# Attention and two dense stages in fp32r on one core: the key blocks of the row maximum, from 384, 384, 384 to 512, 512, 128 columns

## The reference

```python
def _attn_ref(q, k, v):
    B, H, S, D = q.shape                      # 4, 8, 1152, 64
    q_pool = q.reshape(B, H, S // 2, 2, D).mean(axis=3)
    scores = 1.0 / np.sqrt(D) * np.matmul(q_pool, k.transpose(0, 1, 3, 2))
    scores = scores - np.max(scores, axis=-1, keepdims=True)
    attn = np.exp(scores)
    attn = attn / (np.sum(attn, axis=-1, keepdims=True) + 1e-09)
    return np.matmul(attn, v)

def _moe_ref(x, w_in, w_out):                 # 512 -> 2048 -> 512
    h = x @ w_in
    return (h * (1.0 / (1.0 + np.exp(-h)))) @ w_out

def _moe2_ref(x, w1, w2, w3, w_out):          # 512 -> 1024 -> 1024 -> 512
    return (((x @ w1) * (x @ w2)) @ w3) @ w_out
```

## Time and profile before

| | us |
|---|---|
| median of 3 runs | 1342.31 |
| the profiled execution | 1341.67 |
| its span in the trace | 1339.6 |
| TensorE busy | 1292.4 (96%) |
| VectorE busy | 592.4 (44%) |
| ScalarE busy | 599.6 (45%) |
| GpSimd busy | 342.5 (26%) |

### The profile page before, as it was taken

The page is one execution under the profiler, slowest core; times in us unless marked ns, Lnnn a source line. Parts: engine busy times, 40 slices in busy tenths (PEclk is TensorE's granted clock), DMA queues, the critical chain, the costliest instruction groups (busy, mean ns, idle before and its releaser), DMA issues.

```text
span 1339.6 us, 26046 instructions
## 1 busy us (share of the span) xinstructions
PE 1292.4 (96%) x10896; PEld 1151.2 (86%) x10896; DVE 592.4 (44%) x886; ACT 599.6 (45%) x1114; POOL 342.5 (26%) x295
## 2 busy tenths in 40 slices
PE   6999999999999999999999999999999999999998
PEld 4999999999999999988888888888998888888888
DVE  6777777777767777733311112111136222222221
ACT  3666666667666666673322222222245121212211
POOL 4556565665656565440000000000000000000000
PEclk9999999999999999999999999999999999999999
DMA  4122222221121211102100000000125000000001
GB/s 136 47 70 71 72 71 72 72 71 49 60 72 54 71 58 50 36 27 64 48 8 1 1 0 1 0 0 0 48 88 180 0 1 32 0 32 0 32 9 40
DMA packets 25300, 58.57 MB, mean 44 GB/s; under 512 B 7136, under 2 KB 7776, under 8 KB 25184
## 3 DMA queue, kind: packets, MB, share of 16 engines
q1 hardware_dynamic: 25184, 56.91, 13.2%
HBM read 52.04 MB, written 4.79 MB: 42 GB/s over the span
## 4 chain that ended last, share of the span: by engine, by line
PE 91%; DVE 3%; ACT 3%; issue 2%; DMA 1%; POOL 0%; ACTq 0%; SPq 0%; DVEq 0%
PE psum L875 18%; PE psum L877 18%; PE psum L876 18%; PE psum L942 17%; PE psum L892 9%; PE psum L921 8%; PE psum L923 2%; DVE mx L682 2%; ACT psum L501 1%; DVE pL L716 1%; ACT tmpB L517 1%; PE psum L903 1%; ACT tmpA L516 1%; ACT qH L522 0%; DMA qraw<-in_qT 0%
## 5 line engine op out<-in xcount | busy, mean ns | idle before, releaser
L682 DVE TENSOR_REDUCE mx<-psum 128x2 f32<-128x768 f32 x240 | 228.6, 957 | 95.8 <-PE psum L892 95.8
L496 ACT ACTIVATE pH<-psum 128x576 fp32r<-128x576 f32 x288 | 188.5, 655 | 179.9 <-PE psum L923 178.9
L942 PE MATMUL psum<-pH,vH 64*128 64x288 f32 x1152 | 196.1, 305 | 25.4 <-ACT tmpB L517 23.2
L421 POOL TENSOR_TENSOR pL<-pF,pH 128x576 fp32r<-128x576 f32 x96 | 137.0, 1427 | 227.3 <-ACT pF L499 227.3
L942 PE MATMUL psum<-pH,vL 64*128 64x288 f32 x1152 | 189.1, 292 | 0.0
L942 PE MATMUL psum<-pL,vH 64*128 64x288 f32 x1152 | 188.7, 291 | 0.0
L812 DVE TENSOR_TENSOR gL<-gF,gH 128x512 fp32r<-128x512 f32 (+1 forms) x80 | 51.4, 642 | 305.2 <-ACT gH L587 305.2
L716 DVE TENSOR_TENSOR pL<-psum,pH 128x576 fp32r<-128x576 f32 x192 | 144.5, 752 | 70.6 <-ACT psum L501 69.1
L584 ACT ACTIVATE gF<-psum 128x512 f32<-128x512 f32 (+1 forms) x80 | 44.4, 555 | 266.8 <-PE psum L877 265.5
L942 PEld LDWEIGHTS psum<-pH,vH 64*128 64x128 f32 x1152 | 127.2, 184 | 41.0 <-issue 30.9
L942 PEld LDWEIGHTS psum<-pH,vL 64*128 64x128 f32 x1152 | 127.4, 185 | 0.0
(11 more groups left out here) (96 smaller groups left out, 2702.5 us busy)
## 6 DMA issues: line engine op xcount, KB each, us to landing
qraw<-in_qT SPq DMA_DIRECT2D x16, 576.0 KB, 4.7
kraw<-in_kT SPq DMA_DIRECT2D x16, 576.0 KB, 3.7
vraw<-in_v SPq DMA_DIRECT2D x16, 576.0 KB, 3.8
rsums<-recips SPq DMA_DIRECT2D x32, 144.0 KB, 3.0
wstage<-in_w_in SPq DMA_DIRECT2D x16, 256.0 KB, 4.7
fstage<-in_w3T SPq DMA_DIRECT2D x8, 512.0 KB, 4.9
w12stage<-in_w SPq DMA_DIRECT2D x8, 512.0 KB, 4.6
outT<-oS SPq DMA_DIRECT2D x4, 1024.0 KB, 4.2
```

The costliest lines, as they stand in the source:

```text
L421: pool.tensor_tensor(pL[r][:], pF[n // 3 % 2][:], pH[r][:].bitcast(F32), ALU.subtract).then_inc(pL_pool, 1)
L496: act.activation(pH[r][:], scores, ACT.Exp, scale=SCALE).then_inc(pH_ready, 1)
L682: dve.tensor_reduce(mx[:, qt, :, kb], bank[:, :, 0:KW], AX.X, ALU.max).then_inc(max_taken, 1)
L942: last = pe.matmul(obank[hd], vals[own(rows_of), c, hd:hd + 2, :].rearrange("p e d -> p (e d)"), probs[own(rows_of), hd, :], start=(c == 0 ...
```

## The change

The key blocks become 0 to 511, 512 to 1023 and 1024 to 1151. Items of key blocks 0 and 1 have matmuls of 512 columns, which fill a PSUM bank, and one reduction over 2 x 512 elements. Items of key block 2 have 128 columns and 2 x 128 elements. The order of items and units, and the cut of v, stay. The splits `k_hi` and `k_lo` get the same widths, and the unit they wait for moves from 12, 15, 18 to 13, 17, 18 done of the pair two before.

```diff
-    KW = S // KB
+    KEDGE = (0, 512, 1024, S)
...
         def kblock(b):
-            return slice(b * KW, (b + 1) * KW)
+            return slice(KEDGE[b], KEDGE[b + 1])
+
+        def kwidth(b):
+            return KEDGE[b + 1] - KEDGE[b]
...
             def k_lo(p, b):
                 pool.wait_ge(kH_ready, KB * p + b + 1)
-                need(pool, st_scored, 2 * (UNITS * (p - 2) + NC + CPB * (b + 1)))
+                need(pool, st_scored, 2 * (UNITS * (p - 2) + NC + KEDGE[b + 1] // P))
...
             def k_hi(p, b):
                 act.wait_ge(k_loaded, 16 * (p + 1))
-                need(act, st_scored, 2 * (UNITS * (p - 2) + NC + CPB * (b + 1)))
+                need(act, st_scored, 2 * (UNITS * (p - 2) + NC + KEDGE[b + 1] // P))
...
-                dve.tensor_reduce(mx[:, qt, :, kb], bank[:, :, 0:KW], AX.X, ALU.max).then_inc(max_taken, 1)
+                dve.tensor_reduce(mx[:, qt, :, kb], bank[:, :, 0:kwidth(kb)], AX.X, ALU.max).then_inc(max_taken, 1)
...
-                        last = pe.matmul(bank[:, hd, 0:KW], q[j][own(hd), cols], k[j][own(hd), keys],
+                        last = pe.matmul(bank[:, hd, 0:kwidth(kb)], q[j][own(hd), cols], k[j][own(hd), keys],
                                          start=(s == 0), stop=(s == 2))
```

More of the change, by code:

```diff
@@ L62, in block_kernel @@
     RING = 4
-    assert NC == 9 and Q <= 1024 and KW <= 512 and ITEMS == QT * KB == 15
+    assert NC == 9 and Q <= 1024 and ITEMS == QT * KB == 15
     TILE = 512
```

## The result

The changed kernel takes 1374.11 us (median of 4 runs, 1373.85 to 1374.30) against 1342.70 us (4 runs) beside it: a ratio of 1.0232, 95% interval 1.0214 to 1.0249. It is slower. The forecast was 1375 with a range of 1356 to 1391. The profiled execution's span went from 1339.6 to 1372.2 us, 32.6 more.

A forecast was written before the change was run, and what follows sets the result against it. TensorE bounds it, through a slackless item-reduction-item loop. Per round 2.98 + 0.34 - 1.56 + 0.35 = 2.11 us, by 15 rounds 31.7, plus 1.1 at the start: 1374.4 profiled, so 1375; range 1356 to 1391.

The forecast's parts named there:

- The loop: Item, reduction, item through one pair of PSUM banks sets wide steps: 2.37 us against TensorE's own 2.04.
- The seven loops: Steps after wide items 0, 3, 6, 7, 9, 12 and 13, set by bank reuse: together +2.98 us a round.
- Items with room behind: Wide items with a gap behind: items 1 and 10 pay only columns, +0.17 us each; item 2, before a stall, 0.
- Narrow items: Steps after 128-column items 4, 5 and 8 shorten by 0.28, 0.34 and 0.29 us; item 11, before a stall, 0.
- the reading of `turn_max`: Its nine 64-column matmuls were taken as 0.042 us each, so a 128-column pair was priced at 0.084 us.
- After item 14: `score_t` 16 starts 2.11 us after narrow item 14 in place of 2.76, its low part coming sooner: -0.65 a round.
- The cast: ScalarE's cast of key block 1 runs ahead of exponential 16, delaying item 0: +0.35 us a round, ends 0 and +0.6.
- The start: Pair 0: longer first block, VectorE waits once, about 0.5 us: +1.1 us, between 0.3 and 2.
- rival 1: Waits are absorbed and TensorE pays only columns: +0.35 us a round, 1347 us; chance 0.07.
- rival 2: Faster: wide reductions end within TensorE's own step of 2.04 us, round -0.25, 1338 us; chance 0.04.
- rival 3: Narrow matmuls are dear: a 128-column pair takes 0.21 us, +23 us, 1398 us; chance 0.06.
- rival 4: TensorE's clock falls to half for 3.3 us in each round, costing 25 us: 1400 us; chance 0.03.

The follow-up runs named there:

- the first experiment: The changed kernel, but VectorE reduces only the first 384 columns of each bank of a wide item, matmuls untouched: 1346.88 us, ratio to before 1.0025.

## Why the prediction was right

**The loop.** The mechanism held and the first experiment shows it: with the reduction back at 0.96 us and all matmuls as changed, the kernel is 27 us faster. The seven loops measured +2.71 us a round against the forecast +2.98. I had added to every wide item the 0.83 us lead of an item that had waited. The lead is 0.92 where the first pair was prompt (309.41 to 310.33) and 1.00 where it waited (311.70 to 312.70), so loops that follow a free item are 2.29, not 2.37.

**Items with room behind.** Item 1 +0.17 and item 2 +0.01, as forecast. Items 10 and 11 +0.25 against +0.17. The difference is item 10's first pair: 0.17 us before, when nothing held it, and 0.305 after, 0.07 more than a wide pair costs (0.23), because its bank now comes free late. With the shorter reduction of the first experiment that pair is back at 0.23 and the step 0.07 shorter.

**Narrow items.** This term was mis-sized: the three steps after items 4, 5 and 8 gave 0.68 against 0.91.

The step of the prediction that failed is the reading of `turn_max`. Its 0.38 us for nine matmuls is not an even 0.042 each: in the trace's records the first two pairs start 0.03 us apart (311.75 and 311.78) and the next ones 0.11 apart (311.89, 312.00, 312.11). So a pair of 64 columns costs 0.11 as well, and a pair of 128 costs 0.115 (314.20 to 314.32 to 314.43), not 0.084. The first pair of a narrow item is quick when nothing held it (0.06 in item 5) and takes 0.13 after a wait, and the first `values` pair behind a narrow item takes 0.18 to 0.20 in place of 0.13 (medians). In all, three narrow pairs cost 0.34 us, and 0.41 after a wait, against the 0.25 and 0.32 forecast: the missing 0.08 or so an item.

The 256-column pairs at 0.12 show that this price is nearly flat from 64 to 256 columns. It follows the clock: at a granted clock of 0.50 the pairs of `turn_max` stand 0.21 apart, and its nine matmuls, which before took 0.64 us from first start to last end at 1.00, took 1.24:

```profile
24.82 1.24 PE L906 MATMUL psum<-identR,mneg 64*128 64x64 f32 x9 [2.46 <-DVE mneg L702]
```

The prediction set beside this the estimate of 0.21 us for two weight loads one behind the other, from the Trainium skill's page "TensorE: Matmul & The Clock Gate", section "LDWEIGHTS (loading the stationary operand)". As a sum of two loads it was wrong here, for the loads of the two halves run beside each other (311.86 and 311.88, each 0.19 us long). But the prediction was also wrong to say that the trace disagrees with the page. The 0.042 us is a mean over the loads of both halves, and the page's estimate of 107 ns for one load of 128 columns is close to the 0.11 us that the trace shows between two matmuls of the same half, each with its own load, at full clock. At half clock the same distance is 0.21.

**After item 14.** -0.72 in place of -0.65. `score_t` 16 lost its wait, as forecast, at 2.13 against 2.11; the rest came from its own first pair, which no longer follows a wait (0.53 to `turn_max` in place of 0.63). The narrow last item put in the kernel before shows this gain by itself: 7 us.

**The cast.** +0.27 in place of +0.35, within its ends, and shown from both sides: 3.9 us when it is moved in the changed kernel, 3.7 us when only the split is changed in the old one (0.3 of it in the start). The 0.27 was the part that I had let through to item 0. Before, nothing held item 0 (its first pair took 0.17, and the placing copy had ended 0.37 earlier), so part of the exponential's delay of 0.48 was absorbed. The 0.08 for a slow first pair was counted twice: it does not move item 0's start but shows in the step behind it (2.40, that of an item that waited), and the 2.37 of that step held it already.

**The start** was too low: +1.52 to the first `turn_max` against +1.1. The first reduction came 0.70 later and VectorE waited once, for 0.48, both as forecast:

```profile
9.82 5.72 DVE L685 TENSOR_REDUCE mx<-psum 128x2 f32<-128x1024 f32 x6 [3.03 <-PE psum L895]
16.02 7.87 DVE L685 TENSOR_REDUCE mx<-psum 128x2 f32<-128x1024 f32 x9 [0.48 <-PE psum L895]
```

The other 0.34 is that the 15 reductions fill 13.59 us in place of 13.25. The first wide items start 1.28 us apart (9.55, 10.83, 12.11, 13.39), with pairs 0.43 apart in place of 0.23, slower than VectorE reduces them.

**The first round** cost 1.0 more than the others, which the prediction did not hold at all. There items 0, 1 and 2 stand nearly side by side, and the loops are bare (0 to 1 2.33 to 2.92, 1 to 2 1.95 to 2.68). The lower clock is the likely cause of that 1.0. It lasted longer here, until 31.3 us, where before it ended at 28.0. The first two lines are of the changed kernel, the third is of the kernel before:

```profile
24.90:28.20 3.30, 2.69 (x20) 2.52 (x22) 0.42 (x1) 0.65 (x3) 0.00 (x0) 0.50 0.02 5
28.05:31.30 3.25, 2.79 (x18) 2.21 (x18) 1.23 (x1) 2.39 (x5) 1.82 (x2) 0.50 0.00 0
28.05:31.30 3.25, 2.09 (x24) 1.80 (x26) 2.09 (x3) 1.39 (x3) 2.33 (x3) 1.00 0.18 44
```

The kernel with the cast moved had 0.50 only from 26.7 to 30.1 in its profiled execution; its first round is 36.70 us, 1.96 over before, where its other rounds are 1.72 over. The one with the shorter reduction had it from 23.8 to 34.1, and its first round is 2.26 over before, where the others are 0.28 over. Whether the longer stretch belongs to the change or to the execution is not shown.

The start's 0.4 and this 1.0 cancel the 1.5 us by which fourteen rounds fell short of the forecast, so the total of +32.6 against +32.8 is closer than the terms deserve. That much of it is luck.

**The rivals.** Waits were not absorbed (rival 1) and wide steps did not come down to 2.05 (rival 2) until the reduction was shortened. The seven loops of rival 2 add up to 0.95, not 0.97, which changes nothing. Narrow pairs cost 0.115, above my value and far below the 0.21 of rival 3. The clock (rival 4) fell once behind the start, as before but for longer, and not again in the rounds:

```profile
60.00:600.00 540.00, 511.53 (x6498) 468.58 (x6500) 364.75 (x542) 348.40 (x664) 298.74 (x251) 1.00 0.19 59
```

With six waits of some 0.26 us in each round the granted clock stays at 1.00, the 2.4 GHz level, from 60 to 600 us.

## What to carry to other kernels

When a producer and a consumer share one buffer, add up the whole loop (write, hand over, read, hand back) and set it against the work that the producer has in between. As long as the loop is shorter, the consumer's time for a piece is free, and only the producer's own work on it counts; above it every nanosecond of both counts. It follows, though no run here tried it, that equal pieces are best where the work between them is equal. Where it is not, as here around the stalls of units 1, 2, 10 and 11, give the large pieces to the places with room and the small one to the end that a long chain waits for: that made this kernel 0.9% faster (1331.3 us).

A change of a block's size can also move a wait's number without moving an instruction. Look at what the new number asks for and what stands behind it in that engine's queue: here it was 4 us of the 31.

## What the runs showed of the hardware

Matmul pairs on the two halves of the rows, started back to back with a new weight load each, stand apart by 0.23 us at 512 columns, 0.175 at 384, 0.13 at 288, 0.12 at 256 and 0.115 at 128. With 64 columns (`turn_max`) it is 0.11, once the first two pairs are past; the 0.084 of the prediction is a mean over them. At a granted clock of 0.50 it is 0.21 there. A price that is the same from 64 to about 256 columns and doubles at half clock is neither one of columns nor a fixed time. Each of these pairs loads new weights of 128 columns in each half; that this load sets the floor fits, but no run changed it, so it is not shown.

A VectorE reduction out of PSUM took 0.42, 0.82, 0.96 and 1.22 us for 256, 640, 768 and 1024 elements a partition, a straight line of 1.04 ns per element with 0.16 us ahead of it.

The first matmul pair after a semaphore wait that was met late took 0.25 us in place of 0.175 at 384 columns, and 0.31 in place of 0.23 at 512, a loss of 0.08 that no idle row of the profile shows.
